# A fused two-stage attention and two feed-forward layers on one core: the 576 keys cut into pieces of 116 and 112 rows in place of 128 and 64

## The reference

```python
p_packed = sm_attn(p, k, v)              # batch 8, heads 8: 32 packed queries, 576 keys, head size 64
out      = sm_attn(q, p_packed, p_packed)
x   = out as (4608 tokens, 512)
x   = prelu(x @ w_in, alpha) @ w_out     # 512 -> 2048 -> 512
out = (silu(x @ w_gate) * (x @ w_val)) @ w_down   # 512 -> 1536 -> 512
```

## Time and profile before

| | |
|---|---|
| median of 3 runs | 1561.51 us (1561.45 to 1562.32) |
| span of the profiled execution | 1558.5 us |
| PE busy | 1551.1 us, 9330 matmuls |
| DVE, ACT, POOL busy | 1110.4, 710.9, 176.1 us |
| chain that ended last | PE 93%, DVE 5%, ACT 1%, DMA 1%, issue 1% |

### The profile page before, as it was taken

The page is one execution under the profiler, slowest core; times in us unless marked ns, Lnnn a source line. Parts: engine busy times, 40 slices in busy tenths (PEclk is TensorE's granted clock), DMA queues, the critical chain, the costliest instruction groups (busy, mean ns, idle before and its releaser), DMA issues.

```text
span 1558.5 us, 24848 instructions
## 1 busy us (share of the span) xinstructions
PE 1551.1 (100%) x9330; PEld 1435.2 (92%) x9330; DVE 1110.4 (71%) x1954; ACT 710.9 (46%) x1426; POOL 176.1 (11%) x193
## 2 busy tenths in 40 slices
PE   9999999999999999999999999999999999999999
PEld 6999999999999999999988888888888889999999
DVE  5565669877888789888755686557765685677666
ACT  4665567555765557655522252124422251234223
POOL 2654441000000010024200000000000000000000
PEclk9999999999999999999999999999999999999999
DMA  8444223442543345358566666676676667887865
GB/s 274 127 127 118 88 82 108 141 127 81 167 132 130 105 163 172 108 186 291 178 238 211 221 214 198 223 254 206 175 241 223 221 201 261 292 284 242 291 231 195
DMA packets 134055, 293.16 MB, mean 188 GB/s; under 512 B 13472, under 2 KB 44208, under 8 KB 133936
## 3 DMA queue, kind: packets, MB, share of 16 engines
q1 hardware_dynamic: 122096, 249.08, 50.4%
q0 software_dynamic: 11840, 42.48, 7.1%
HBM read 239.61 MB, written 51.90 MB: 187 GB/s over the span
## 4 chain that ended last, share of the span: by engine, by line
PE 93%; DVE 5%; ACT 1%; DMA 1%; issue 1%; SPq 0%; DVEq 0%; ACTq 0%
PE acc L1061 13%; PE h L842 10%; PE side L842 9%; PE h L844 9%; PE h L843 9%; PE side L843 9%; PE side L844 9%; PE acc L1065 7%; PE acc L842 5%; PE acc L844 5%; PE acc L843 5%; DVE piece L1521 1%; DVE mixed L1521 1%; DVE floats L1740 1%; PE side L995 1%
## 5 line engine op out<-in xcount | busy, mean ns | idle before, releaser
L1061 PE MATMUL acc<-g,w 128*128 128x288 f32 x1792 | 272.3, 294 | 0.0
L1061 PEld LDWEIGHTS acc<-g,w 128*128 128x128 f32 x1792 | 249.0, 188 | 0.0
L1405 ACT ACTIVATE rows_b<-side 128x512 f32<-128x512 f32 (+1 forms) x60 | 33.4, 556 | 285.6 <-PE side L844 285.6
L1202 ACT ACTIVATE g<-floats 128x288 fp32r<-128x288 f32 x192 | 85.3, 444 | 165.1 <-DVE floats L1740 120.4
L842 PE MATMUL h<-attn,mixed 128*128 128x288 f32 x512 | 156.6, 306 | 0.6 <-DVE g L1521 0.5
L1065 PE MATMUL acc<-g,w 128*128 128x288 f32 x896 | 156.1, 296 | 0.0
L844 PE MATMUL h<-attn,mixed 128*128 128x288 f32 x512 | 151.0, 295 | 0.0
L843 PE MATMUL h<-attn,mixed 128*128 128x288 f32 x512 | 150.9, 295 | 0.0
L1065 PEld LDWEIGHTS acc<-g,w 128*128 128x128 f32 x896 | 131.2, 188 | 0.0
L1202 ACT ACTIVATE piece<-floats 128x512 fp32r<-128x512 f32 (+3 forms) x217 | 128.9, 616 | 3.6 <-PE side L844 2.9
L1521 DVE TENSOR_TENSOR g<-floats,g 128x288 fp32r<-128x288 f32 x192 | 87.4, 455 | 50.0 <-ACT g L1202 48.7
(11 more groups left out here) (319 smaller groups left out, 3931.5 us busy)
## 6 DMA issues: line engine op xcount, KB each, us to landing
ring<-w_scratch SPq DMA_DIRECT2D x90, 512.0 KB, 4.6
wring<-d_scratch SPq DMA_DIRECT2D x157, 256.0 KB, 2.9
ring_c<-w_scratch SPq DMA_DIRECT2D x60, 512.0 KB, 3.9
w_scratch<-piece POOLq DMA_DIRECT2D x36, 512.0 KB, 3.7
floats<-w_in SPq DMA_DIRECT2D x64, 256.0 KB, 3.2
ring_b<-w_scratch SPq DMA_DIRECT2D x30, 512.0 KB, 5.1
ring<-d_scratch SPq DMA_DIRECT2D x46, 256.0 KB, 3.0
d_scratch<-piece POOLq DMA_DIRECT2D x42, 256.0 KB, 3.7
```

The lines of the kernel that those rows point to most:

```text
L1061: pe.matmul(acc[:, m, 0:CH], w2[:, j, x, m * P:(m + 1) * P], g[:, s % 2, 0, :], start=False, stop=False)
L1202: return nc.scalar.activation(dst, src, ACT.Copy, **kw)
```

## The change

A constant `KT = 116` is added. Piece t now has keys 116t to 116t + 115, the last keys 464 to 575, which are 112. `rows(t)` is partitions 0 to 115, and 0 to 111 for the last. The number of pieces stays 5, and so does the order of all steps. The transposes now take just the keys of their piece and write as many partitions. The loads of v take 116 and 112 rows. ACT's copy in `turned_0` covers 116 partitions.

```diff
+KT = 116
...
         def rows(t):
-            return slice(max(0, (t + 1) * P - SEQ), P)
+            return slice(0, min(KT, SEQ - t * KT))
 
         def keys(t):
-            return slice(min(t * P, SEQ - P), min((t + 1) * P, SEQ))
+            return slice(t * KT, min((t + 1) * KT, SEQ))
...
                 elif p[0] == "v":
                     dst = dst[rows(p[2]), :]
-                    src = vS[p[1], p[2] * P:min((p[2] + 1) * P, SEQ), :]
+                    src = vS[p[1], keys(p[2]), :]
...
             for t in range(ST):
-                sp.dma_start(v0[rows(t), t, :], vS[0, t * P:min((t + 1) * P, SEQ), :]).then_inc(v0_landed, 16)
+                sp.dma_start(v0[rows(t), t, :], vS[0, keys(t), :]).then_inc(v0_landed, 16)
...
                 for t in range(ST):
-                    mm = pe.transpose(acc[:, 2 * half + t // 4, t % 4 * P:(t % 4 + 1) * P], s1[:, half, keys(t)], ident)
+                    mm = pe.transpose(acc[rows(t), 2 * half + t // 4, t % 4 * P:(t % 4 + 1) * P],
+                                      s1[:, half, keys(t)], ident)
...
                 for half in range(2):
-                    mm = pe.transpose(side[:, 0, half * P:(half + 1) * P], s1[:, half, keys(t)], ident)
+                    mm = pe.transpose(side[rows(t), 0, half * P:(half + 1) * P], s1[:, half, keys(t)], ident)
...
                 once.wait_ge(t1_done, half + 1)
-                copy(probs0[:, 0:4, half * P:(half + 1) * P], acc[:, 2 * half, :].rearrange("p (t n) -> p t n", t=4)
+                k = rows(0)
+                copy(probs0[k, 0:4, half * P:(half + 1) * P], acc[k, 2 * half, :].rearrange("p (t n) -> p t n", t=4)
```

## The result

The changed kernel takes 1570.65 us, the median of 5 runs (1569.66 to 1571.12), against 1561.51 before; the ratio is 1.0054, 95% interval 1.0043 to 1.0066, which is 6.7 to 10.3 us. It is slower, in the way that was forecast, and the time lies in the range; the forecast of 6.3 us was too small.

What follows compares the result with a forecast made beforehand. PE, busy for all of the span, was taken as the bound. 7.4 + 2.1 + 0.8 - 3.5 - 0.5 = 6.3 us more, from 1561.5 to 1567.8 us; range 1558 to 1572.5.

Steps and rivals of the forecast that it cites:

- equal shares on the same 4 engines: Loads of v: each 116-row transfer runs on the same first four DMA engines, 29 rows each; 10.3 us of moves hang on it.
- rival A: Loads of v: unequal shares, all 16 engines with 7 or 8 rows, no loss; 1557.5 us, chance 0.12.
- rival B: Loads of v: equal shares moving to the next four engines, only batch 1 late; 1558.3 us, chance 0.06.
- The start: Batch 0: v lands at 18.4 us and not 10.98, so PE's work from packed_0 on shifts by 7.4 us.
- The clock: PE behind its new idle time at the start: some 4.2 us at half speed, costing 2.1 us; bounds 0 and 4.2.
- Batch 1: ACT's copies of v come late, delaying g for PE's matmuls at 73.87 us; 0.8 us lost, bounds 0 and 2.5.
- The 64-row form: PE's piece 4 products: no switch into and out of 64 rows, 3.5 us gained over all batches; bounds 0 and 3.5.
- Rival D: Piece 4's product: 112 rows keep a form of their own, no switch saved; 1571.3 us, chance 0.05.
- The transposes: PE's 80 transposes load 116 columns as weights and not 128; 0.5 us gained, between 0 and 0.8.
- Batches 2 to 7: Loads of v there: soonest read 10.6 us after issue against 4.4 needed, so hidden by the four raw places; no cost.

Runs made afterwards that it cites:

- v alone: Changed kernel, but SP waits until all of v has landed before it issues q and w_in; 1567.81 us, ratio 1.0034.
- the four other kernels with a late start: Changed kernel with v alone, with q after w_in, with w_in alone beside v, or with 128-row loads in batches 1 to 7; 1567.81, 1571.09, 1571.41, 1569.25 us.
- the same change by itself: Kernel before, but piece 4 gets all 128 rows in products and loads of v (result wrong); 1557.51 us, ratio 0.9974.

## Why the prediction was right, and where its sizes were off

The step on which it hung, equal shares on the same 4 engines, held: 384 notices fewer, and PE's first matmul on v 9.95 us later. The notices rule out rival A alone; the landing rules out A and rival B, which would both have had it at 11 us. The total was 2.9 us off, and its terms missed both ways. The range, 14.5 us wide, would have held rival B as well, so the time alone would have proved little.

*The start, 7.4 us.* This is the term that was mis-sized: it measured 9.95. The 87 rows more were priced at 0.085 us each, taken from a stretch in which all 16 engines were at work on the same transfers. With v alone that price holds (17.53 us, 18.4 forecast). Beside other transfers v lands at 20.5 to 21.4 us, 3.0 to 3.9 us later, which over 123 rows is 0.025 to 0.03 us more for each: some 0.11 us a row, an estimate. I had assumed that the other 12 engines don't matter to the four.

*The clock, 2.1 us.* It fell, as expected, and in the profiled execution cost 1.46 us: it was back 3.1 us after PE's restart and not 4.2. In the four other kernels with a late start and nothing to fill it, it cost 2.0 to 3.1 us. So 2.1 is a fair size, and one execution does not tell it to 1 us.

*Batch 1, 0.8 us.* 0.9 us, but not at the matmuls that were named, and the nearness is luck. PE's matmuls at 73.87 do not read the g that ACT copies at 73.15: their counterparts start at 84.57 us, before that copy starts at 85.66, and are no later than the rest. PE waits at the next product on v, for DVE's low part of `pp`. There 1.07 us were to spare and not 0.3. Against this, ACT's first wait was longer than forecast (1.97 us, not 1.2). Of it, 0.17 was an idle time that ACT had there before, so 1.97 - 0.17 - 1.07 = 0.73 should reach PE. Its product starts 86.95 - 75.46 - 10.70 = 0.79 late, and the step to the next matmul takes 0.22 us and not 0.11: together 0.9. By the same count a wait of 1.02 costs nothing, as the kernel with 128 rows at the start shows. The second wait was shorter than forecast, 0.49 us.

*The 64-row form, -3.5 us.* -0.78 in batch 0 as forecast, and about -2.6 in the seven other batches where 2.7 was forecast; the same change by itself is worth 0.26% (0.17 to 0.36), 2.7 to 5.6 us. Rival D falls.

*The transposes, -0.5 us.* Nothing: five of 116 columns take 0.55 us, as five of 128.

*Batches 2 to 7.* No wait for v is left in the trace of the changed kernel after batch 1: hidden, as forecast.

The terms as measured, 9.95 + 1.46 + 0.9 - 0.8 - 2.6 = 8.9 us, stand against 9.1 us between the medians and 8.4 by the ratio. The clock in this sum is that of one execution. The 10.4 us between the two profiled spans have these 1.0 to 1.4 us of the end in them.

## What to carry to other kernels

A cut is also a choice of transfer shape: check how the rows of a piece divide over the DMA engines before counting what it saves on PE. Here pieces of 116 rows cost 11 us at the start, and pieces of 112 and 128 keep the 3 us of gain. A product on 64 rows between products on 128 costs 0.4 us in and out, which one on 112 rows does not. And to say what a late copy costs, follow it to the instruction that reads its result: here it was another than the one that stood next in time.

## What was not expected of the hardware

Four DMA engines with a transfer of their own took longer when the other twelve had work: v landed at 17.53 us alone, at 20.54 beside transfers of 2 KB rows and at 20.66 to 21.38 beside q and w_in. The core then moved 245 to 255 GB/s with its engines busy for 0.89 to 0.98 of the time, against 387.

And the issuing is held up. SP's issue of the five transfers of v took 5.13 us in the changed kernel, and of the first eight of w_in 7.61 us. In the kernel before they took 2.48 and 4.09, and with the 128-row loads 2.60 and 3.86. SP's timeline of the changed kernel:

```profile
3.07 5.13 SPq L677 DMA_DIRECT2D early<-vS  x5
8.25 1.97 SPq L668 DMA_DIRECT2D early<-qT  x2
10.26 7.61 SPq L663 DMA_DIRECT2D early<-w_in  x8
```

So transfers that use few engines also held back the issue of those behind them that use all 16. That a queue fills would explain it, but no view shows the queue.

The clock did not come back at a fixed time. Behind 10.2 to 10.8 us of idle time PE's work ran at the lower level for 3.1 us in one execution and for more than 5 us in another.
